# Fused attention, mixture of experts and MLP: the start and the end of the MLP rearranged

## The chip, the cores and the metric

One core of one Trainium2 chip. The metric is the device time of one execution, in microseconds (us); lower is better.

## The reference

Windowed and dilated attention, then a mixture of eight experts with one expert for each row, then an MLP whose activation is `h * cos(h)`. What is cut away here is the attention and the gate's softmax.

```python
def _moe_ref(x, expert_emb, tau, w1, w2):          # N = 2304, D = 512, E = 8, F = 1024
    ...                                            # expert_idx, gate_w: arg max and softmax of cosine logits
    for e in range(E):
        mask = expert_idx == e
        h = np.maximum(x[mask] @ w1[e], 0.0)
        out[mask] = gate_w[mask, None] * (h @ w2[e])

def _moe2_ref(x, w_in, w_out):                     # 512 -> 2048 -> 512
    h = x @ w_in
    g = h * np.cos(h)
    return (g @ w_out).astype(np.float32)
```

## The kernel before, in words

**Splitting.** Every matrix product of the experts and of the MLP is made of three passes (`passes`, L698): each operand is split into a high part, a rounded copy made by ScalarE, and a low part, the difference, made by VectorE, and TensorE adds high by low, low by high and high by high. So each weight tile costs ScalarE one copy (`weights_hi`, L912, L920) and VectorE one subtraction (`weights_lo`, L1222, L1227), and so do the input rows and the hidden layer.

**Experts.** The rows lie sorted by expert in `XS`; a block is up to 352 rows of one expert, with `nblk` blocks (8 with these inputs, at most 14). A block has eight units `f` (128 hidden columns each). For each unit TensorE does `expert_up(f)` (12 matmuls) and then `expert_dn` of two units before (12 matmuls), so units 6 and 7 of a block are brought down in the first units of the next (`expert_block`, L745). ScalarE's block (L978) takes each unit with a Relu (L986), converts weights of the next pair of units, at units 5 and 6 the next block's rows (L951), and at unit 6 the first pair of the next block's weights. Its `expert_dn_hi` at unit 6 waits until TensorE has done unit 5's down product, and unit 7's Relu stands behind it. In the last block (L1008 and L1397) that is skipped by an `If`. Blocks 0 to 5 are written out on all engines (`FLAT`); the rest are a `Fori` over pairs of blocks with an `If` for each (L766, L1017, L1408), which runs to block 13 and skips those that are not there. SyncE loads weights two pairs ahead (`load_expert`, L359), into two raw buffers for each of the two weights.

**Handing over to the MLP.** TensorE has left the loop and brings down units 6 and 7 of the last block, with `mlp_up(0, 0)` between them and `mlp_up(0, 1)` behind. SyncE waits until all expert weights are converted (L399) and then loads the first MLP weights (L407, L409). ScalarE converts `w_in` pair 0 as two halves, the input rows 0 to 383 in one instruction (`group_hi(0, 0)`, L1024, four row tiles of 128x384), `w_out` pair 0, rows 384 to 767, and then runs a Sin on two columns, which loads the sine table (L1076). VectorE makes the low parts in the same order (L1416 for rows). `mlp_up(m, i)` (L775) waits for the whole of the low rows. The rows buffers `yh`, `yl` share memory with the experts' `XS`.

**MLP.** Three groups `m` of 768 rows, each of two halves of 384; 32 units a group, a unit being one hidden tile `f` for one half; `unit_of` (L771) gives their order: two `f` of half 0, the same two of half 1. TensorE does `mlp_up(m, i)` (12 matmuls of 384 columns), then `mlp_dn(m, i - 2)` (9 of 512, into three banks for each half). Between them stands a chain over two engines: ScalarE `turns` (L1039), VectorE three steps (`reduce`, L1428 to L1433), ScalarE Abs and Sin (L1051, L1054), VectorE the gate (L1445), ScalarE the high part (L1045), VectorE the low part (`gated_lo`, L1438), which `mlp_dn` needs. At units 29 and 31 each engine also converts the rows of the next group's half 0 and half 1 in one instruction (L1024, L1416); on VectorE `group_lo` stands ahead of `gated_lo`. `group_out` (L1056, L1447) copies a half's three banks out (ScalarE the even ones, VectorE the odd ones) once the last down product of that half is done; half 0 at unit 31 behind the cosine or the gate, half 1 at unit 1 of the next group. GpSimd sends each copied tile to its rows of `out` by an indirect DMA (L526). The program ends when all have landed.

Of the kernel before, what the change touches and what calls it, by code (L numbers as in the profile page):

```python
# [5 lines left out]
ALU = mybir.AluOpType  # L6
# [7 lines left out]
P = 128  # L14
# [7 lines left out]
def fused_kernel(nc, q, k, v, emb, tau, w1, w2, w_in, w_out, out):  # L22
# [36 lines left out]
    FLAT = 6  # L59
    FIRST_INC = (1, 1, DT - 2)  # L60
    IDENT_STEPS, MASK_STEPS, CONSTS = 2, 6, 18
# [5 lines left out]
    with ExitStack() as ctx:  # L67
# [11 lines left out]
        half_pi = sb("half_pi", [P, 2])  # L79

# [157 lines left out]
        def weight_sems(p, units):  # L238

            return dict(  # L240
                up_in=[sem(f"{p}_up_in{i}") for i in range(2)], dn_in=[sem(f"{p}_dn_in{i}") for i in range(2)],
                up_hi=sem(f"{p}_up_hi"), up_lo=sem_from(f"{p}_up_lo", 2),
                dn_hi=sem(f"{p}_dn_hi"), dn_lo=sem_from(f"{p}_dn_lo", 2),
                up_mm=sem_from(f"{p}_up_mm", units), dn_mm=sem_from(f"{p}_dn_mm", units),
                in_hi=sem(f"{p}_in_hi"), in_lo=sem(f"{p}_in_lo"))
        ex = weight_sems("ex", 4)
        ml = weight_sems("ml", 8)
# [4 lines left out]
        table_loaded = sem("table_loaded")  # L252
        turns_ready = sem("turns_ready")
# [66 lines left out]
        def _(sp):  # L320
# [212 lines left out]
        def _(pe):  # L533
# [237 lines left out]
            def unit_of(i):  # L771

                return i // 4 * 2 + i % 2, i % 4 // 2

            def mlp_up(m, i):  # L775

                f, half = unit_of(i)
# [7 lines left out]
                for d in range(DT):  # L785
                    last = passes(bank[6 + i % 2][:, 0:HR], (up_h[s][:, d, cols], up_l[s][:, d, cols]),
                                  (yh[half][:, d, :], yl[half][:, d, :]), d == 0, d == DT - 1)
                last.then_inc(ml["up_mm"], 1)

            def mlp_dn(m, i):  # L790
# [6 lines left out]
                if i % 4 == 0:  # L797
                    pe.wait_ge(ml["dn_lo"], m * PAIRSTEPS2 + i // 4 + 3)
                i %= 2 * FT2
                f, half = unit_of(i)  # L800
                s = f // 2 % 2
                for c in range(3):
                    if f == 0:
# [5 lines left out]
                                  (dn_h[s][:, f % 2, :], dn_l[s][:, f % 2, :]), f == 0, f == FT2 - 1)  # L809
                last.then_inc(ml["dn_mm"], 1)  # L810
# [30 lines left out]
        def _(act):  # L841
# [136 lines left out]
            def expert_block(i, u, nblk):  # L978
# [3 lines left out]
                for f in range(FT):  # L982
# [73 lines left out]
            def group_out(m, half):  # L1056

                act.wait_ge(ml["dn_mm"], m * 2 * FT2 + (6 + 2 * half))
                act.wait_ge(o_free, m)
                for c in range(3 * half, 3 * half + 3):  # L1060
                    if c % 2 == 0:
# [10 lines left out]
            group_hi(0, 0)  # L1072
            act.wait_ge(ex["dn_mm"], nblk * FT + 2)
# [445 lines left out]
```

## Time and profile before

| | us |
|---|---|
| median of 3 runs | 874.77 (874.3 to 877.12) |
| the profiled execution, its own time | 870.1 |
| its span, first to last instruction | 868.4 |
| TensorE busy | 832.7 (96% of the span) |
| VectorE busy | 604.4 (70%) |
| ScalarE busy | 481.7 (55%) |
| TensorE's mean granted clock | 0.991 of full speed |

In the profile a step on TensorE appears as a matmul instruction with its start and modelled length; these lengths overlap, so the pace is read from one start to the next. "Idle before" in brackets is the time that the engine stood still before an instruction, with what ended it.

### The profile page before, as it was taken

The numbers are of one execution on the slowest core, as the hardware profiler recorded it, in microseconds if no ns is written. First come the engines' busy times: TensorE is split into PE (matmuls) and PEld (weight loads), VectorE is DVE, ScalarE is ACT, GpSimd is POOL, SyncE is SP. The second block draws the span as 40 slices with busy tenths as digits, with TensorE's granted clock in tenths as the row PEclk, the third lists the DMA queues.
The fourth block names the chain that finished last, engine by engine and source line by source line (L and its number), as shares of the span: only waits on it lengthen the run. The fifth ranks groups of instructions, "written<-read, shape, count | busy, mean of one in ns | idle before, by whom it ended". The sixth has DMA issues, their size and how long they took to land.

```text
span 868.4 us, 15558 instructions
## 1 busy us (share of the span) xinstructions
PE 832.7 (96%) x5034; PEld 757.4 (87%) x5034; DVE 604.4 (70%) x1157; ACT 481.7 (55%) x920; POOL 74.8 (9%) x129
## 2 busy tenths in 40 slices
PE   7999999979999999999989999999999999999993
PEld 6778876769999999999988999989999988999992
DVE  7888886676556556555567777788777788777762
ACT  4567764334445544454456665676666676566651
POOL 3112112141101000000000000002000002000002
PEclk9999999999999999999999999999999999999998
DMA  6597887035454343434242112113211214122001
GB/s 146 137 215 177 195 188 208 27 110 164 153 169 157 125 144 123 145 122 146 74 146 74 53 69 73 49 66 129 74 61 61 73 49 146 49 73 73 2 0 74
DMA packets 114912, 93.78 MB, mean 108 GB/s; under 512 B 65816, under 2 KB 94488, under 8 KB 114848
## 3 DMA queue, kind: packets, MB, share of 16 engines
q1 hardware_dynamic: 109920, 78.81, 31.4%
q0 software_dynamic: 4928, 14.16, 4.9%
q8 instruction: 35, 0.57, 0.3%
q14 instruction: 29, 0.24, 0.1%
HBM read 83.51 MB, written 9.44 MB: 107 GB/s over the span
## 4 chain that ended last, share of the span: by engine, by line
PE 83%; DVE 8%; ACT 2%; issue 2%; DMA 2%; POOL 1%; DVEq 0%; ACTq 0%; SPq 0%; POOLq 0%
PE bank L700 24%; PE bank L702 24%; PE bank L701 24%; PE bank L588 2%; PE bank L567 2%; PE bank L641 2%; PE bank L576 1%; PE bank L551 1%; DVE shifted L1168 1%; DVE row_max L1165 1%; DVE yl L1416 1%; ACT probs L869 1%; DMA xtok<-x_rows 1%; PE bank L657 1%; PE bank L742 1%
## 5 line engine op out<-in xcount | busy, mean ns | idle before, releaser
L700 PE MATMUL bank<-yh,up_l 128*128 128x384 f32 x384 | 129.7, 338 | 2.3 <-DVE yl L1416 2.3
L702 PE MATMUL bank<-yh,up_h 128*128 128x384 f32 x384 | 129.9, 338 | 0.0
L701 PE MATMUL bank<-yl,up_h 128*128 128x384 f32 x384 | 129.3, 337 | 0.0
L700 PE MATMUL bank<-dn_h,hid 128*128 128x512 f32 x288 | 112.7, 391 | 2.3 <-DVE hid L1438 1.8
L702 PE MATMUL bank<-dn_h,hid 128*128 128x512 f32 x288 | 113.9, 396 | 0.0
L701 PE MATMUL bank<-dn_l,hid 128*128 128x512 f32 x288 | 113.7, 395 | 0.0
L1227 DVE TENSOR_TENSOR dn_l<-dn_raw,dn_h 128x512 fp32r<-128x512 f32 (+1 forms) x80 | 71.9, 900 | 51.8 <-ACT dn_h L920 51.8
L1039 ACT ACTIVATE work<-bank 128x384 f32<-128x384 f32 x96 | 47.2, 492 | 80.4 <-PE bank L702 80.4
L700 PE MATMUL bank<-xh,up_l 128*128 128x352 f32 x256 | 83.9, 328 | 3.7 <-DVE up_l L1227 3.0
L1051 ACT ACTIVATE work<-work 128x384 f32<-128x384 f32 x96 | 50.4, 525 | 64.8 <-DVE work L1433 64.8
L1428 DVE TENSOR_SCALAR work<-work 128x384 f32<-128x384 f32 x96 | 34.5, 360 | 72.7 <-ACT work L1039 72.4
L920 ACT ACTIVATE dn_h<-dn_raw 128x512 fp32r<-128x512 f32 (+1 forms) x80 | 63.7, 798 | 37.7 <-PE bank L702 37.7
L700 PE MATMUL bank<-hid,dn_l 128*128 128x352 f32 x256 | 83.0, 324 | 0.8 <-issue 0.8
L701 PE MATMUL bank<-hid,dn_h 128*128 128x352 f32 x256 | 83.0, 324 | 0.0
L702 PE MATMUL bank<-hid,dn_h 128*128 128x352 f32 x256 | 82.6, 323 | 0.0
L702 PE MATMUL bank<-xh,up_h 128*128 128x352 f32 x256 | 82.3, 322 | 0.0
L701 PE MATMUL bank<-xl,up_h 128*128 128x352 f32 x256 | 82.0, 320 | 0.0
L1227 DVE TENSOR_TENSOR up_l<-up_raw,up_h 128x512 fp32r<-128x512 f32 (+1 forms) x80 | 71.9, 900 | 11.3 <-ACT up_h L920 10.7
L700 PEld LDWEIGHTS bank<-yh,up_l 128*128 128x128 f32 x384 | 72.3, 188 | 6.8 <-DVE yl L1416 2.6
L986 ACT ACTIVATE hid<-bank 128x352 fp32r<-128x352 f32 x64 | 29.7, 464 | 84.6 <-PE bank L702 84.2
L701 PEld LDWEIGHTS bank<-yl,up_h 128*128 128x128 f32 x384 | 72.3, 188 | 4.0
L702 PEld LDWEIGHTS bank<-yh,up_h 128*128 128x128 f32 x384 | 72.3, 188 | 0.0
(195 smaller groups left out, 1683.0 us busy)
## 6 DMA issues: line engine op xcount, KB each, us to landing
up_raw<-in_moe_w_dram SPq DMA_DIRECT2D x32, 512.0 KB, 3.6
dn_raw<-in_moe_w_dram SPq DMA_DIRECT2D x32, 512.0 KB, 3.5
up_raw<-in_moe_w_in_dram SPq DMA_DIRECT2D x24, 512.0 KB, 3.4
dn_raw<-in_moe_w_out_dram SPq DMA_DIRECT2D x24, 512.0 KB, 3.4
qn<-in_q_dram SPq DMA_DIRECT2D x32, 144.0 KB, 2.8
kn<-in_k_dram SPq DMA_DIRECT2D x32, 144.0 KB, 3.2
xtok<-x_rows SPq DMA_DIRECT2D x4, 1152.0 KB, 7.6
x_rows<-osb POOLq DMA_DIRECT2D x8, 288.0 KB, 3.6
```

Of the source, the lines that this page charges most:

```text
L567: last = mm(o[:QT, i * 256:(i + 1) * 256].rearrange("p (h c) -> p h c", h=2), qT[p % 2][:, t * QT:(t + 1) * QT], kT[p % 2][:, :, t * QT:t ...
L588: last = mm(bank[6 + s % 2][:QT, i * VN:(i + 1) * VN], probsT[s % 2][:, i * QT:(i + 1) * QT], vw[p % 2][:, 2 * u + i // 2, i % 2, :], star ...
L641: last = mm(bank[4 + G % 2][:E, 0:2 * QT], embT[:, d, :], xT[G % 2][:, d, :], start=d == 0, stop=d == DT - 1)
L700: mm(o, w[1], x[0], start=first, stop=False, skip_group_check=True)
L701: mm(o, w[0], x[1], start=False, stop=False, skip_group_check=True)
L702: return mm(o, w[0], x[0], start=False, stop=last, skip_group_check=True)
L920: A(hi[s][:, rows, :], raw[s][:, rows, :], ACT.Copy).then_inc(w[f"{which}_hi"], 1)
L986: A(hid[:, f % 4, 0, 0:TB], bank[4 + f % 4][:, 0:TB], ACT.Relu).then_inc(ex_h_hi, 1)
L1039: A(turns, bank[6 + i % 2][:, 0:HR], ACT.Copy, scale=1 / (2 * PI), bias=ROUND).then_inc(turns_ready, 1)
L1051: A(folded, red2, ACT.Abs).then_inc(folded_ready, 1)
L1227: ins = tt(lo[s][:, rows, :], raw[s][:, rows, :], hi[s][:, rows, :], ALU.subtract)
L1428: ts(whole, turns, ROUND, None, ALU.subtract).then_inc(whole_ready, 1)
```

## The change

The first pair of MLP weights is loaded and converted as if it belonged to the next expert (semaphores of `ex`), inside the last expert block. ScalarE and VectorE have all eight sure blocks written out, with the loop behind one `If(nblk > SURE)`. The first half's rows are converted in four pieces with a signal each. The sine table is loaded ahead of block 4. `group_lo` of later groups is split in two halves over units 29, 30, 31 and 0. In the last group the order of the last eight units is a list, and output tiles are signalled one by one (`chunk_mm`). SyncE's loop over groups is written out. The diff, cut to its core:

```diff
+    TRIG_BLOCK = 4
+    LAST_UNITS = ((12, 0), (13, 0), (12, 1), (14, 0), (15, 0), (13, 1), (14, 1), (15, 1))
...
-            sp.wait_ge(ex["up_lo"], nblk * PAIRSTEPS + 2)
-            sp.wait_ge(ex["dn_lo"], nblk * PAIRSTEPS + 2)
-            sp.sem_inc(carrier, 1)
...
-            with sp.Fori(0, NM) as m:
-                for j in range(PAIRSTEPS2):
+            for j in range(2):
+                sp.wait_ge(ex["up_lo"], nblk * PAIRSTEPS + (j + 1))
+                sp.dma_start(up_raw[j][:], win_v[:, :, 256 * j:256 * j + 256]).then_inc((ex, ml)[j]["up_in"][j], 16)
+                sp.wait_ge(ex["dn_lo"], nblk * PAIRSTEPS + (j + 1))
+                sp.dma_start(dn_raw[j][:], wout_v[:, 2 * j:2 * j + 2, :]).then_inc((ex, ml)[j]["dn_in"][j], 16)
+            sp.wait_ge(ex["up_lo"], nblk * PAIRSTEPS + 3)
+            sp.wait_ge(ex["dn_lo"], nblk * PAIRSTEPS + 3)
+            for m in range(NM):
+                for j in range(0 if m else 2, PAIRSTEPS2):
...
-            def unit_of(i):
+            def unit_of(m, i):
+                if m == NM - 1 and i >= 2 * FT2 - len(LAST_UNITS):
+                    return LAST_UNITS[i - 2 * FT2 + len(LAST_UNITS)]
                 return i // 4 * 2 + i % 2, i % 4 // 2
             def mlp_up(m, i):
...
-                if f == 0:
+                if f == 0 and (m, i) != (0, 0):
                     pe.wait_ge(ml["in_lo"], m * 2 + half + 1)
-                if i % 4 == 0:
-                    pe.wait_ge(ml["up_lo"], m * PAIRSTEPS2 + i // 4 + 3)
+                if (m, i) == (0, 0):
+                    pe.wait_ge(ex["up_lo"], nblk * PAIRSTEPS + 3)
+                elif f % 2 == 0:
+                    pe.wait_ge(ml["up_lo"], m * PAIRSTEPS2 + f // 2 + 3)
...
                 for d in range(DT):
+                    if (m, i) == (0, 0):
+                        pe.wait_ge(start_rows_lo, d + 1)
...
+                    if f == FT2 - 1 and c < 2:
+                        last.then_inc(chunk_mm, 1)
                 last.then_inc(ml["dn_mm"], 1)
...
                     elif f == FT - 2:
-                        if sure and b < SURE - 1:
-                            expert_up_hi(i, J)
-                            expert_dn_hi(i, J)
-                        else:
-                            with act.If(i * 2 + (u + 1) < nblk):
-                                expert_up_hi(i, J)
-                                expert_dn_hi(i, J)
+                        expert_up_hi(i, J)
+                        expert_dn_hi(i, J)
...
-            for b in range(1, FLAT):
+            for b in range(1, SURE):
+                if b == TRIG_BLOCK:
+                    A(trig_junk[:], half_pi[:], ACT.Sin).then_inc(trig_loaded, 1)
+                    act.wait_ge(trig_loaded, 1)
                 expert_block(b // 2, b % 2, nblk)
-            with act.Fori(FLAT // 2, NBLK // 2) as i:
-                for u in range(2):
-                    with act.If(i * 2 + u < nblk):
-                        expert_block(i, u, nblk)
+            with act.If(nblk > SURE):
+                with act.Fori(SURE // 2, NBLK // 2) as i:
...
             def group_out(m, half):
-                act.wait_ge(ml["dn_mm"], m * 2 * FT2 + (6 + 2 * half))
                 act.wait_ge(o_free, m)
                 for c in range(3 * half, 3 * half + 3):
+                    if c % 3 < 2:
+                        act.wait_ge(chunk_mm, (m - 1) * 4 + 2 * half + c % 3 + 1)
+                    else:
+                        act.wait_ge(ml["dn_mm"], m * 2 * FT2 + (6 + 2 * half - (m == NM and half == 0)))
                     if c % 2 == 0:
                         A(osb2[:, c, :], bank[c][:], ACT.Copy).then_inc(o_out_a, 1)
-            act.wait_ge(ex["up_lo"], nblk * PAIRSTEPS + 2)
-            act.wait_ge(ex["up_mm"], nblk * FT + 4)
-            whole_weights_hi("up", up_raw, up_h)
             act.wait_ge(y_out_a, nblk * 2)
             act.wait_ge(y_out_d, nblk * 2)
             act.wait_ge(ex["in_lo"], nblk * DT + DT)
-            group_hi(0, 0)
-            act.wait_ge(ex["dn_mm"], nblk * FT + 2)
-            whole_weights_hi("dn", dn_raw, dn_h)
+            for d in range(DT):
+                A(yh[0][:, d, :], X[:, d, 0:HR], ACT.Copy).then_inc(start_rows_hi, 1)
             group_hi(0, 1)
-            A(folded[:, 0:2], half_pi[:], ACT.Sin).then_inc(table_loaded, 1)
-            act.wait_ge(table_loaded, 2)
...
+                    if m == NM - 1 and i == 2 * FT2 - 1:
+                        group_out(NM, 0)
                     act_cosine(m, i)
...
-                    if i == 2 * FT2 - 1:
+                    if i == 2 * FT2 - 1 and m < NM - 1:
                         group_out(m + 1, 0)
...
-            for part in range(2):
-                weights_lo(ml, "up", up_raw, up_h, up_l, part + 1, 2, part)
-            group_lo(0, 0)
-            for part in range(2):
-                weights_lo(ml, "dn", dn_raw, dn_h, dn_l, part + 1, 2, part)
+            for d in range(DT):
+                dve.wait_ge(start_rows_hi, d + 1)
+                tt(yl[0][:, d, :], X[:, d, 0:HR], yh[0][:, d, :], ALU.subtract).then_inc(start_rows_lo, 1)
             group_lo(0, 1)
...
-                    if i in (2 * FT2 - 3, 2 * FT2 - 1):
-                        if m < NM - 1:
-                            group_lo(m + 1, (i - 2 * FT2 + 3) // 2)
+                    if i >= 2 * FT2 - 3 and m < NM - 1:
+                        group_lo(m + 1, (i - 2 * FT2 + 3) // 2, (i - 2 * FT2 + 3) % 2, 2)
+                    if i == 0 and m > 0:
+                        group_lo(m, 1, 1, 2)
```

VectorE's expert blocks, its `group_out` and the place of the last `group_out(NM, 0)` (ahead of `gate`) change as ScalarE's do.

## Rows read from the trace of the kernel before

**Rows 1.** The page: the span.

```profile
span 868.4 us, 15558 instructions
```

**Rows 2.** Waits of TensorE over the whole run: engine, line, releaser: us, times, longest.

```profile
PE bank L700 <- DVE yl L1416: 2.3, 1, 2.3
```

**Rows 3.** Timeline of TensorE, 408 to 457 us: start us, us, engine, line, op, operands.

```profile
409.49 0.32 PE L702 MATMUL bank<-hid,dn_h 128*128 128x352 f32 x1
...
440.11 0.32 PE L702 MATMUL bank<-hid,dn_h 128*128 128x352 f32 x1
...
441.21 0.42 PE L700 MATMUL bank<-hid,dn_l 128*128 128x352 f32 x1 [0.78 <-issue]
...
443.07 0.32 PE L702 MATMUL bank<-hid,dn_h 128*128 128x352 f32 x1
...
445.73 0.44 PE L700 MATMUL bank<-yh,up_l 128*128 128x384 f32 x1 [2.34 <-DVE yl L1416]
...
456.67 0.47 PE L700 MATMUL bank<-dn_h,hid 128*128 128x512 f32 x1 [0.94 <-DVE hid L1438]
```

**Rows 4.** Stretches: us, length, busy of each engine (instructions), PEclk, DMA share, GB/s.

```profile
194.00:196.00 2.00, 0.14 (x1) 0.14 (x2) 1.85 (x3) 0.95 (x2) 0.00 (x0) 1.00 0.00 0
...
447.00:448.00 1.00, 1.00 (x5) 1.00 (x4) 1.00 (x1) 0.80 (x2) 0.00 (x0) 0.50 0.04 12
```

**Rows 5.** Timeline of ScalarE, 318 to 447 us.

```profile
318.51 0.47 ACT L986 ACTIVATE hid<-bank 128x352 fp32r<-128x352 f32 x1 [0.45 <-PE bank L702]
...
409.91 1.06 ACT L920 ACTIVATE dn_h<-dn_raw 128x1024 fp32r<-128x1024 f32 x1 [3.62 <-PE bank L702]
...
410.88 0.45 ACT L986 ACTIVATE hid<-bank 128x352 fp32r<-128x352 f32 x1
...
441.36 1.15 ACT L920 ACTIVATE up_h<-up_raw 128x512 fp32r<-128x512 f32 x2 [2.34 <-issue]
...
446.32 1.28 ACT L1076 ACT_TABLE_LOAD   x1
```

**Rows 6.** Timeline of VectorE, 408 to 456 us.

```profile
412.14 0.95 DVE L1380 SCALAR_TENSOR_TENSOR hid<-bank,hid 128x352 fp32r<-128x352 f32 x2
...
426.31 1.23 DVE L1227 TENSOR_TENSOR dn_l<-dn_raw,dn_h 128x1024 fp32r<-128x1024 f32 x1 [2.04 <-ACT dn_h L920]
...
446.80 1.75 DVE L1416 TENSOR_TENSOR yl<-X,yh 128x1536 fp32r<-128x1536 f32 x1
...
449.49 0.36 DVE L1428 TENSOR_SCALAR work<-work 128x384 f32<-128x384 f32 x1 [0.94 <-ACT work L1039]
...
454.21 0.36 DVE L1428 TENSOR_SCALAR work<-work 128x384 f32<-128x384 f32 x1 [0.52 <-ACT work L1039]
```

**Rows 7.** Timeline of TensorE and VectorE, units 27 of group 0 to 1 of group 1.

```profile
565.60 0.39 PE L700 MATMUL bank<-dn_h,hid 128*128 128x512 f32 x1
...
569.79 0.39 PE L700 MATMUL bank<-dn_h,hid 128*128 128x512 f32 x1
...
571.97 1.75 DVE L1416 TENSOR_TENSOR yl<-X,yh 128x1536 fp32r<-128x1536 f32 x1
...
591.44 0.39 PE L700 MATMUL bank<-dn_h,hid 128*128 128x512 f32 x1
```

**Rows 8.** Timeline of TensorE, VectorE and GpSimd, the last output tiles.

```profile
853.02 0.50 PE L700 MATMUL bank<-dn_h,hid 128*128 128x512 f32 x1 [0.36 <-DVE hid L1438]
...
855.40 1.29 DVE L1453 COPY osb<-bank 128x512 f32<-128x512 f32 x2 [2.43 <-PE bank L702]
...
856.37 0.97 POOL L526 DMA_INDIRECT out_dram<-osb,id_now  x1 [1.09 <-DVE osb L1453]
...
858.92 0.97 POOL L526 DMA_INDIRECT out_dram<-osb,id_now  x1 [0.30 <-issue]
```

**Rows 9.** The page: a queue's packets, MB, share; an issue's count, KB, us to landing.

```profile
q8 instruction: 35, 0.57, 0.3%
...
dn_raw<-in_moe_w_out_dram SPq DMA_DIRECT2D x24, 512.0 KB, 3.4
```

More of the change, by code:

```diff
@@ L236, in fused_kernel, with weight_sems @@
         carrier = sem("carrier")
-        def weight_sems(p, units):
+        def weight_sems(p, units, rows=0):
+            if not rows:
+                pairs = dict(up_in=[sem(f"{p}_up_in{i}") for i in range(2)], dn_in=[sem(f"{p}_dn_in{i}") for i in range(2)],
+                             up_hi=sem(f"{p}_up_hi"), up_lo=sem_from(f"{p}_up_lo", 2),
+                             dn_hi=sem(f"{p}_dn_hi"), dn_lo=sem_from(f"{p}_dn_lo", 2))
+            else:
+                pairs = dict(up_in=[sem_from(f"{p}_up_in0", 16), sem(f"{p}_up_in1")],
+                             dn_in=[sem_from(f"{p}_dn_in0", 16), sem(f"{p}_dn_in1")],
+                             up_hi=sem_from(f"{p}_up_hi", 2), up_lo=sem_from(f"{p}_up_lo", 3),
+                             dn_hi=sem_from(f"{p}_dn_hi", 2), dn_lo=sem_from(f"{p}_dn_lo", 3))
             return dict(
-                up_in=[sem(f"{p}_up_in{i}") for i in range(2)], dn_in=[sem(f"{p}_dn_in{i}") for i in range(2)],
-                up_hi=sem(f"{p}_up_hi"), up_lo=sem_from(f"{p}_up_lo", 2),
-                dn_hi=sem(f"{p}_dn_hi"), dn_lo=sem_from(f"{p}_dn_lo", 2),
+                **pairs,
                 up_mm=sem_from(f"{p}_up_mm", units), dn_mm=sem_from(f"{p}_dn_mm", units),
-                in_hi=sem(f"{p}_in_hi"), in_lo=sem(f"{p}_in_lo"))
+                in_hi=sem_from(f"{p}_in_hi", rows) if rows else sem(f"{p}_in_hi"),
+                in_lo=sem_from(f"{p}_in_lo", rows) if rows else sem(f"{p}_in_lo"))
         ex = weight_sems("ex", 4)
-        ml = weight_sems("ml", 8)
+        ml = weight_sems("ml", 8, 1)
+        start_rows_hi = sem("start_rows_hi")
+        start_rows_lo = sem("start_rows_lo")
+        chunk_mm = sem("chunk_mm")
         ex_h_hi = sem("ex_h_hi")
@@ L252, in fused_kernel @@
         table_loaded = sem("table_loaded")
+        trig_loaded = sem("trig_loaded")
         turns_ready = sem("turns_ready")
@@ L1392, in expert_block @@
                     elif f == FT - 2:
-                        if sure and b < SURE - 1:
-                            expert_up_lo(i, J)
-                            expert_dn_lo(i, J)
-                        else:
-                            with dve.If(i * 2 + (u + 1) < nblk):
-                                expert_up_lo(i, J)
-                                expert_dn_lo(i, J)
+                        expert_up_lo(i, J)
+                        expert_dn_lo(i, J)
                     if sure and tile_at(b, f) is not None:
@@ L1405, in _, with group_lo @@
             last_start = dve.value_load(table[0:1, 1, bass.ds(nblk, 1)], min_val=0, max_val=N)
-            for b in range(FLAT):
+            for b in range(SURE):
                 expert_block(b // 2, b % 2, nblk)
-            with dve.Fori(FLAT // 2, NBLK // 2) as i:
-                for u in range(2):
-                    with dve.If(i * 2 + u < nblk):
-                        expert_block(i, u, nblk)
-            def group_lo(m, half):
+            with dve.If(nblk > SURE):
+                with dve.Fori(SURE // 2, NBLK // 2) as i:
+                    for u in range(2):
+                        with dve.If(i * 2 + u < nblk):
+                            expert_block(i, u, nblk)
+            def group_lo(m, half, part=0, parts=1):
                 dve.wait_ge(ml["in_hi"], m * 2 + half + 1)
-                tt(yl[half][:], X[:, :, bass.ds(m * MR + half * HR, HR)], yh[half][:], ALU.subtract).then_inc(ml["in_lo"], 1)
+                ds_ = slice(part * DT // parts, (part + 1) * DT // parts)
+                ins = tt(yl[half][:, ds_, :], X[:, ds_, bass.ds(m * MR + half * HR, HR)], yh[half][:, ds_, :], ALU.subtract)
+                if part == parts - 1:
+                    ins.then_inc(ml["in_lo"], 1)
             def mlp_weights_lo(m, i):
@@ L1483, in _ @@
                             mlp_weights_lo(m, i)
+                    if m == NM - 1 and i == 2 * FT2 - 1:
+                        group_out(NM, 0)
                     gate(m, i)
@@ L1489, in _ @@
                         before_this(dve, m, lambda: group_out(m, 1))
-                    if i == 2 * FT2 - 1:
+                    if i == 2 * FT2 - 1 and m < NM - 1:
                         group_out(m + 1, 0)
```

20 lines of the change are left out of this document (15 added, 5 removed).

## The prediction

> **What bounds the kernel now.** I read the page first: the span is 868.4 us [rows 1], and TensorE is the engine that is busy nearly throughout, so only time in which it stands still, or runs slower, can be won. The profiled execution took 870.1 us, 1.7 more than its span; the median of the runs shown is 874.77, so 4.7 more than the execution that I reason from. What those 4.7 are, no row tells. I take differences from the profile and set them on the median.
>
> Then the view of TensorE's waits: the longest inside the MLP is for the low rows `yl`, 2.3 us, once [rows 2]. The timeline of TensorE shows the place, the hand-over from the last expert block to the MLP [rows 3]. The last matmul of block 7's down unit 5 starts at 440.11; unit 6 starts at 441.21 (0.78 idle, "issue": the loop's skipped blocks); it is through at about 443.23 (443.07 and a pace of 0.16); `mlp_up(0, 0)` starts at 445.73, behind a wait for `yl`; `mlp_dn(0, 0)` starts at 456.67, behind another 0.94 for the low part of the hidden layer. In between TensorE fell from 2.4 to 1.2 GHz: granted clock 0.50 from 447 to 448 [rows 4]. That loss is in the pace of the matmuls, not in a wait. A stretch of 2 us with 0.14 us of matmuls (194 to 196) kept 1.00 [rows 4], so idle time here does not always bring the clock down.
>
> Next, why `yl` was late. ScalarE's next step behind its last Relu began at 441.36, after 2.34 us of "issue" [rows 5]: it ran through three passes of the loop with six tests, all not taken. Only then came weights, rows, weights, rows, and the table load at 446.32, 1.28 long [rows 5]. VectorE followed it: second row instruction at 446.80 (1.75), first step of the first unit at 449.49, first step of the second at 454.21, of which 0.52 was a wait that goes back to TensorE's half clock [rows 6].
>
> Two more places. The start of the down products runs at 4.19 us a unit (565.60 to 569.79), but from 565.60 to 591.44 six units take 25.84, where six times 4.19 are 25.14 [rows 7]: 0.70 lost at the border of two groups, where VectorE has the 1.75 us of `yl` (571.97) ahead of `gated_lo`. The other border has the same pattern, so there are two. And the end: last down unit from 853.02, first copy of half 1 at 855.40, the last three scatters at 856.37 to 858.92, one each 1.27 (0.97 and 0.30 of issue), then 8.5 us to the end of the span [rows 8].
>
> **The change, part by part. Hand-over.** SyncE's loads of MLP pair 0 move ahead: `w_out` pair 0 waits for the low part of pair 2 of block 7, which ends at 427.54 (426.31 + 1.23) [rows 6], and lands 3.4 later [rows 9], about 431. Its loads are queued behind each other as an expert's are, and nothing else stands behind them. ScalarE now converts `up` pair 0 in the slack of unit 6, and `dn` pair 0 when unit 5's down product is done; the Relu of unit 7 is queued behind that. Block 6 shows how long this takes: last matmul of unit 5 at 409.49, conversion 409.91, Relu 410.88 [rows 3, 5], VectorE's low part of unit 7 as the first of a pair from 412.14 (0.95 for two, so 0.48 a step) [rows 6]. Set on 440.11 this gives conversion 440.53, Relu 441.50 to 441.95, low part 442.76 to about 443.25. So the Relu waits for a conversion that the old last block did not have, but unit 7's down product is not started before `mlp_up(0, 0)` is over, so TensorE does not feel it.
>
> Behind it stand one test and branch over the loop on each engine. No row shows it alone. Bounds: 0, since VectorE ran two Relu halves of different blocks back to back across such a test at 412.14 [rows 6]; and 2.34, the whole loop on ScalarE [rows 5]. I take 0.4, that is 2.34 / 6. The first low row tile then runs from 443.65 to 444.2, and `mlp_up(0, 0)` starts at 444.3, not 445.73: 1.4 earlier. It needs a tile each 0.52 us (three matmuls), VectorE gives one each 0.48, so the four signals cost nothing after the first.
>
> But TensorE is not what sets the end of this stretch; VectorE's chain is. Four tiles end at 445.6, the rows of half 1 take 1.7, and the first step of unit 0 starts at about 447.3 (before: 449.49), 2.2 earlier. `mlp_up(0, 0)` is over by 446.4, in time. From there the chain to `mlp_dn(0, 0)` is the old one, less the 0.52 of waiting for half-clock matmuls, if the clock stays: 2.7 earlier at 456.67. **Term 1: 2.7 us**, bounds 1.2 (half clock again, or a slow branch) and 3.4 (branch free). I expect the clock to stay, because the idle time between unit 6 and `mlp_up` falls from 2.5 to about 1 us. The 0.78 of TensorE's own loop stays.
>
> **Sine table.** 1.28 and a short Sin move from 446.32 to the front of block 4. There ScalarE stood idle 0.45 before the Relu at 318.51 [rows 5], so that Relu and the weight copy behind it come about 1.1 late. The hidden unit is needed two units, some 7.6 us, later, the weights one unit pair later, so this costs nothing; without that cover it would be 1.1. What it saves is in term 1: at the new pace ScalarE would be in the load when `turns` is due. After the load at 446.32 Copy and Abs ran with no second load; no row shows a Relu behind a sine load. The Trainium skill, "ScalarE: Activation LUTs", section "Table sets: the hidden batching unit", says that relu, copy and abs are in every set as filler; by it no further load comes.
>
> **Written-out blocks.** ScalarE and VectorE have slack in blocks 6 and 7 and TensorE's loop is unchanged: nothing gained but the loop's 2.34, counted above. The unrolled SyncE loop issues the same loads: nothing.
>
> **Borders.** `yl` in halves: 0.85 instead of 1.7 ahead of `gated_lo` at units 29 to 31 and 0. The low part of unit 28 then ends about 0.85 before its old time, and TensorE lost only half of the 0.70 there. At unit 0 the half instruction is new, but `gated_lo` of unit 31 is due a whole product later than it can be done. **Term 2: 2 x 0.70, of which I take 1.3**; bounds 0 and 1.4.
>
> **Tail.** With the new list half 0 finishes one unit earlier and is copied ahead of the last cosine, so its three scatters leave by about 853.3. The last gate no longer has ScalarE's two copies between it and the high part: the last down unit starts up to 0.2 earlier, 852.8. Its first third is done at about 853.8, the copy 0.7 later at 854.5, the scatters at 854.8, 856.0 and 857.3 instead of 858.92. The three issues at 1.27 are the limit, and the 8.5 us behind the last remain. The weights for the moved unit (14, 0) are converted at unit 25, three units before it. **Term 3: 1.6 us**; bounds 0.5 and 1.8.
>
> Sum: 2.7 + 1.3 + 1.6 = 5.6. On the profiled execution 870.1 - 5.6 = 864.5; on the median 874.77 - 5.6 = 869.2.
>
> **Rivals.**
> (a) The hand-over gives only 1.2: the branch costs up to 2.34, or the clock falls again, since the stretch still has 0.9 us of issue and about 1 of wait. For it: the fall at 447 came behind two such gaps. Against it: 194 to 196. Total 1.2 + 1.3 + 1.6 = 4.1, so 870.7. One form of it is an instruction fetch behind the jump. The instruction queue moved 35 packets in 0.3% of 16 engines' span [rows 9], 1.2 us each (0.003 x 16 x 868.4 / 35), so a fetch costs at least that. The Trainium skill, "Runtime: NRT & Kernel Launch", section "Instruction fetch mechanics", says that a taken branch to a target outside the pages held forces a fetch before execution goes on; no row here shows one alone.
> (b) Borders and tail give little (another wait takes their place: `yl` of half 1 at unit 0 delays `gated_lo`, or the landing of the last scatter is what ends, not its issue). Then 2.7 + 0 + 0.5 = 3.2, so 871.6; together with (a) 1.7, so 873.1, which is no measurable difference.
> (c) Slower: `w_out` pair 0 comes late. ScalarE's Relu of unit 7 is now queued behind that conversion, so each us after 440.5 is a us of the chain. It decides only if the load lands more than 9 us after the 431 above; to end 2.6 slower it must be some 17 us late. Against it: 24 such loads took 3.4 in the median. Some 877.5.
> (d) The change does nothing at the hand-over because TensorE was bound by its own loop: excluded by the wait for `yl` in rows 2.
>
> **How the numbers follow.** Forecast 0.66, (a) 0.13, (b) 0.12, both together 0.06, (c) 0.03. The forecast's own range is 867.9 to 870.9 (terms at 6.9 and 3.9); 8 in 10 with the median's spread of some 1.5 us gives 866.6 to 872.8. About 0.3%, 2.6 us, is what a measurement of this kernel can tell from no change: faster means below 872.15. Faster: the forecast, (a) and 0.07 of (b), 0.86; same 0.10, the rest of (b) and nearly all of both together; slower 0.04.
>
> **What would show it.** In the changed profile: no 2.34 of issue on ScalarE at the hand-over; `mlp_up(0, 0)` about 1 us after unit 6; granted clock 1.00 from 440 to 460; the table load near 318 with no wait on TensorE behind it; seven down starts over each border at 25.1; last scatter 1.6 earlier to the last gate, and 8.5 us behind it unchanged. Wrong would be: a clock of 0.50 after 444, a second table load, a wait of TensorE for `hid` at the borders, or a longer stretch behind the last scatter.

## The result and the profile after

The changed kernel took 870.60 us (median of 8 runs, 867.19 to 871.85), the kernel before 874.82 on the same chip; the ratio of the fast runs is 0.9938 (95% interval 0.9919 to 0.9957), which stands for 5.4 us, while the two medians lie 4.2 apart. Timed twice more the ratio came to 0.9916 (0.9898 to 0.9935) and 0.9925 (0.9897 to 0.9953). So it is faster, by 4 to 7 us according to the first interval and by up to 9 according to the others. The forecast was 869.2, within 866.6 to 872.8.

The profiled execution took 867.19 us, 2.9 less than the one before. From the page, its span and the busy time of the engines ("to [rows 1]" names the rows of the kernel before that it is to be read against):

```profile
span 865.2 us, 15473 instructions
...
PE 832.7 (96%) x5034; PEld 756.8 (87%) x5034; DVE 604.9 (70%) x1162; ACT 481.7 (56%) x921; POOL 75.9 (9%) x129
```

TensorE's work is the same 832.7 us. Its waits, longest in total first, a choice (to [rows 2]):

```profile
PE bank L719 <- DVE xl L1386: 3.3, 1, 3.3
...
PE bank L719 <- DVE hid L1464: 1.4, 3, 0.6
...
PE bank L719 <- issue: 0.8, 1, 0.8
...
PE bank L719 <- DVE yl L1486: 0.5, 1, 0.5
```

`yl` at the hand-over has fallen from 2.3 to 0.5 us. The 3.3 us for `xl` is in the start of the first expert block and was 0.7 before; it belongs to a stretch that the change does not touch, and the experiments come back to it.

**Hand-over.** TensorE, ScalarE (with the moved table load) and VectorE, in three fences (to [rows 3, 5, 6]):

```profile
442.69 0.32 PE L721 MATMUL bank<-hid,dn_h 128*128 128x352 f32 x1
...
443.79 0.42 PE L719 MATMUL bank<-hid,dn_l 128*128 128x352 f32 x1 [0.78 <-issue]
...
446.47 0.41 PE L719 MATMUL bank<-yh,up_l 128*128 128x384 f32 x1 [0.49 <-DVE yl L1486]
...
455.82 0.47 PE L719 MATMUL bank<-dn_h,hid 128*128 128x512 f32 x1 [0.63 <-DVE hid L1464]
```

```profile
320.66 1.28 ACT L1041 ACT_TABLE_LOAD   x1
...
322.19 0.46 ACT L1015 ACTIVATE hid<-bank 128x352 fp32r<-128x352 f32 x1
...
443.11 1.06 ACT L949 ACTIVATE dn_h<-dn_raw 128x1024 fp32r<-128x1024 f32 x1 [3.62 <-PE bank L721]
...
444.07 0.45 ACT L1015 ACTIVATE hid<-bank 128x352 fp32r<-128x352 f32 x1
...
444.42 1.75 ACT L1101 ACTIVATE yh<-X 128x384 fp32r<-128x384 f32 x4
...
448.83 0.49 ACT L1067 ACTIVATE work<-bank 128x384 f32<-128x384 f32 x1 [1.28 <-PE bank L721]
```

```profile
445.34 0.52 DVE L1407 SCALAR_TENSOR_TENSOR hid<-bank,hid 128x352 fp32r<-128x352 f32 x1
...
445.77 1.96 DVE L1486 TENSOR_TENSOR yl<-X,yh 128x384 fp32r<-128x384 f32 x4
...
449.35 0.36 DVE L1454 TENSOR_SCALAR work<-work 128x384 f32<-128x384 f32 x1
```

ScalarE goes from its last Relu (444.07) into the row tiles (444.42) with no "issue" between, and VectorE from its last low part (445.34) into `yl` (445.77). `mlp_up(0, 0)` starts 3.78 us after the last matmul of block 7's down unit 5, not 5.62, and `mlp_dn(0, 0)` 13.13 after it (442.69 to 455.82), not 16.56. The table load stands ahead of block 4's first Relu, which runs right behind it without another load. The 20 us around the hand-over have the full clock (the column PEclk, third from the end):

```profile
440.00:460.00 20.00, 18.06 (x100) 16.56 (x100) 15.36 (x27) 12.43 (x23) 0.00 (x0) 1.00 0.27 91
```

**Border of two groups.** TensorE's down units 27 and 33 of the MLP (568.92 and 594.33), and up unit 0 and down unit 31 between them (to [rows 7]); then VectorE:

```profile
568.92 0.39 PE L719 MATMUL bank<-dn_h,hid 128*128 128x512 f32 x1
...
583.56 0.33 PE L719 MATMUL bank<-yh,up_l 128*128 128x384 f32 x1
...
585.86 0.50 PE L719 MATMUL bank<-dn_h,hid 128*128 128x512 f32 x1
...
594.33 0.39 PE L719 MATMUL bank<-dn_h,hid 128*128 128x512 f32 x1
```

```profile
584.39 0.95 DVE L1440 TENSOR_TENSOR yl<-X,yh 128x768 fp32r<-128x768 f32 x1
...
585.25 0.55 DVE L1464 TENSOR_TENSOR hid<-work,hid 128x384 fp32r<-128x384 f32 x1
```

Six units take 25.41 us, not 25.83. Six undisturbed ones take 25.14, so 0.27 is left, and it comes from one place: up unit 0 of the new group starts at 583.56 and its twelve matmuls take 2.09, but down unit 31 begins only at 585.86, behind the low part that VectorE wrote from 585.25 to 585.80, and that stood behind the half of `yl` at 584.39.

**Tail.** Last down unit, first copy of half 1, first and last of its three scatters (to [rows 8]):

```profile
851.10 0.50 PE L719 MATMUL bank<-dn_h,hid 128*128 128x512 f32 x1 [0.18 <-DVE hid L1464]
...
852.16 0.69 DVE L1482 COPY osb<-bank 128x512 f32<-128x512 f32 x1 [1.12 <-issue]
...
853.13 0.97 POOL L545 DMA_INDIRECT out_dram<-osb,id_now  x1 [1.24 <-DVE osb L1482]
...
855.69 0.97 POOL L545 DMA_INDIRECT out_dram<-osb,id_now  x1 [0.30 <-issue]
```

The copy starts 1.06 us after the unit, where it was 2.38 before, and the last scatter is at 855.69, 3.5 after that copy in both kernels; 9.5 us to the end of the span behind it, as before.

### The profile page after: what moved, and what is told of

It is laid out like the page before. It is cut to its first block, busy times and chain, and to the rows that moved or that the text cites. A ratio compares the mean times of both kernels' runs of the same rounds, so it can differ in the third digit from the quotient of the medians.

```text
span 865.2 us, 15473 instructions
## 1 busy us (share of the span) xinstructions
PE 832.7 (96%) x5034; PEld 756.8 (87%) x5034; DVE 604.9 (70%) x1162; ACT 481.7 (56%) x921; POOL 75.9 (9%) x129
## 4 chain that ended last, share of the span: by engine, by line
PE 84%; DVE 7%; issue 2%; ACT 2%; DMA 2%; POOL 1%; another core or an unknown queue 0%; DVEq 0%; ACTq 0%; POOLq 0%; SPq 0%
PE bank L721 24%; PE bank L719 24%; PE bank L720 24%; PE bank L607 2%; PE bank L586 2%; PE bank L660 2%; PE bank L595 1%; PE bank L570 1%; DVE shifted L1195 1%; DVE row_max L1192 1%; ACT probs L898 1%; PE bank L676 1%; DMA xtok<-x_rows 1%; DVE kT L319 1%; PE bank L761 1%
```

## Experiments

In all of them I measure three stretches from TensorE's starts in the timeline: the **hand-over**, from the last matmul of block 7's down unit 5 to the first of `mlp_dn(0, 0)`; a **border**, from down unit 27 of a group to down unit 1 of the next (six units), two of them; and the **tail**, from down unit 29 of the last group to the end of the span. The last column is when the hand-over begins. us:

| run | hand-over | borders | tail | begins at |
|---|---|---|---|---|
| before | 16.56 | 25.83, 25.82 | 20.88 | 440.11 |
| e0, before again | 16.48 | 25.86, 25.85 | 20.89 | 448.36 |
| after | 13.13 | 25.41, 25.37 | 19.43 | 442.69 |
| e1, after again | 13.13 | 25.41, 25.36 | 19.43 | 443.97 |
| e8, after, third | 13.13 | 25.41, 25.34 | 19.37 | 442.26 |
| e2, borders whole | 13.13 | 25.85, 25.84 | 19.44 | 446.46 |
| e5, loops back | 15.07 | 25.38, 25.36 | 19.42 | 445.58 |
| e6, sine late | 13.56 | 25.41, 25.36 | 19.42 | 443.49 |
| e7, rows whole | 14.56 | 25.42, 25.36 | 19.40 | 444.48 |
| e3, tail by halves | 13.13 | 25.42, 25.36 | 20.82 | 444.77 |
| e4, tail old | 13.15 | 25.40, 25.36 | 21.04 | 446.25 |
| v8, w_out later | 12.38 | 25.42, 25.36 | 19.37 | 443.19 |
| v9, TensorE's branch | 13.85 | 25.41, 25.36 | 19.46 | 442.03 |
| v12, all | 13.94 | 25.12, 25.12 | 19.42 | 445.01 |

A stretch that an edit does not touch repeats within 0.1 us, while the times of whole executions differ by several us; so parts of 0.4 to 3 us can be told apart here by single profiles. Where a run is named by one time, it is one execution beside one or a few of the kernel before.

**e0, e1, e8: both kernels again.** No edit.

> The kernel before, unchanged, for its profile. Both theories: from the last matmul of block 7's down unit 5 to the first of mlp_dn(0, 0) 16.6 us, six units over a border 25.8, from the start of down unit 29 of the last group to the end 20.9. What is open is the stretch ahead of the experts. Theory: the changed kernel's first expert matmul at 191.47 instead of 188.84 was chance (ScalarE and GpSimd both saw a signal of TensorE 2.7 us late), so the first expert matmul of single runs of either kernel lies anywhere from 188.5 to 192. Rival: the change shifts it, and this one is at 189 again.

> The changed kernel, unchanged. Theory: the three stretches as in its first profile (13.1, 25.4, 19.4 us, against 16.6, 25.8 and 20.9 before), together 5.8 us, and a ratio near 0.9935. Ahead of the experts it is not behind the kernel before by a fixed amount. Rival: the change costs some 2 us ahead of the experts in each run, first expert matmul at 191 or later, which takes back a part of the 5.8, so that the ratio stays near 0.996.

> The changed kernel once more, timed beside v12 on one chip. Both theories: 13.1, 25.4 and 19.4 us in the three stretches, a ratio of 0.991 to 0.994; v12 is under it by 2 us (theory) or by less than 1 (rival).

e0 took 878.86 us; e1 868.38 (median of 5; ratio 0.9916) and e8 866.30 (median of 6; ratio 0.9925). The three stretches came out as in the first profiles. What differs is ahead of them. The first expert matmul starts at 188.84 and 194.87 in the two profiles of the kernel before (e0 thus lies beyond the 188.5 to 192 that was expected) and at 191.47, 189.91 and 188.76 in the three of the changed one, so the changed kernel is not the later one. TensorE's wait for `xl` there is 0.72 in both profiles of the kernel before and 3.31, 1.15 and 0.72 in the changed one, so it varies between executions of one kernel. The hand-over begins at 440.11 and 448.36 in the two profiles of the kernel before and at 442.26 to 443.97 in three of the changed one. The stretches of 20 us around the start of the experts show a good part of it in the clock, column PEclk. e0, with the stretch of the hand-over behind:

```profile
180.00:200.00 20.00, 16.43 (x116) 15.78 (x114) 10.62 (x35) 6.04 (x11) 9.06 (x9) 0.79 0.41 119
...
200.00:220.00 20.00, 18.14 (x107) 18.07 (x108) 10.71 (x14) 7.66 (x13) 4.13 (x4) 0.91 0.53 160
...
440.00:460.00 20.00, 16.90 (x94) 16.33 (x93) 11.91 (x18) 11.00 (x18) 0.00 (x0) 0.91 0.48 159
```

e0 lost 0.21 and 0.09 of 20 us each there, 6 us of full clock; the first profile of the kernel before had 0.98 and 1.00 in the same two stretches, e1 0.92 and 0.99. So the 2.6 us by which the first profile of the changed kernel was behind at the hand-over are within the spread of one and the same kernel; a fixed cost of the change ahead of the experts (the rival) is not seen: the ratio did not stay near 0.996.

**e2: `group_lo` whole at the borders.**

```diff
-                    if i >= 2 * FT2 - 3 and m < NM - 1:
-                        group_lo(m + 1, (i - 2 * FT2 + 3) // 2, (i - 2 * FT2 + 3) % 2, 2)
-                    if i == 0 and m > 0:
-                        group_lo(m, 1, 1, 2)
+                    if i in (2 * FT2 - 3, 2 * FT2 - 1) and m < NM - 1:
+                        group_lo(m + 1, (i - 2 * FT2 + 3) // 2)
```

> VectorE's group_lo in one instruction at units 29 and 31 again, all else as changed. Theory: only the borders move, back from 25.4 to 25.8 us for six units, twice, so 0.85 us longer in all; hand-over 13.1 and tail 19.4 stay. Rival: the borders gained by the other weights and outputs order, and stay at 25.4.

The borders went back to 25.85 and 25.84, the rest stayed. The split alone carries the borders' gain, 0.44 and 0.48 us.

**e5: blocks 6 and 7 in the loop again on ScalarE and VectorE.**

```diff
-            with act.If(nblk > SURE):
-                with act.Fori(SURE // 2, NBLK // 2) as i:
+            with act.Fori(FLAT // 2, NBLK // 2) as i:
...
-            for b in range(1, SURE):
+            for b in range(1, FLAT):
```

and the same on VectorE.

> ScalarE and VectorE have blocks 6 and 7 in the loop again, with no test around it; the weights of MLP pair 0 are still converted in block 7. Theory: ScalarE stands 2.3 us behind its last Relu, the first row tile comes that much later, mlp_up(0, 0) starts some 2.0 us later than in the changed kernel, and the hand-over is 1.5 to 2.3 longer (14.6 to 15.4 us). Rival: the branches are hidden behind the instructions that the engine still has in its queue, as at a test between two blocks, and the hand-over stays at 13.1 to 13.4.

ScalarE stands 1.53 us between its last Relu and the first row tile, not the 2.3 expected (the first fence: its timeline), VectorE 1.83 between its last low part and its first row tile (the second), and `mlp_up(0, 0)` waits 2.42 (the third: TensorE's):

```profile
446.97 0.45 ACT L1015 ACTIVATE hid<-bank 128x352 fp32r<-128x352 f32 x1
...
448.94 1.76 ACT L1100 ACTIVATE yh<-X 128x384 fp32r<-128x384 f32 x4 [1.53 <-issue]
```

```profile
448.23 0.52 DVE L1406 SCALAR_TENSOR_TENSOR hid<-bank,hid 128x352 fp32r<-128x352 f32 x1
...
450.59 1.97 DVE L1484 TENSOR_TENSOR yl<-X,yh 128x384 fp32r<-128x384 f32 x4 [1.83 <-ACT yh L1100]
```

```profile
451.29 0.41 PE L719 MATMUL bank<-yh,up_l 128*128 128x384 f32 x1 [2.42 <-DVE yl L1484]
```

VectorE's wait is put down to ScalarE, but ScalarE's first row tile, one of four in 1.76 us, was over by about 449.5, 1.1 us before VectorE began. So it is mostly VectorE's own loop that holds it: its first row tile starts 5.01 us after the hand-over's start mark (445.58), 1.93 later than in the changed kernel (3.08), and ScalarE's only 1.63 later.

The hand-over is 15.07, 1.94 longer than with the loops behind one test. So the passes through blocks that are not there were on the path, and the one test that replaced them costs nothing that shows. One more thing: with idle pieces of 0.78 and 2.42 us, as long as before, the clock stayed at 1.00 here:

```profile
440.00:460.00 20.00, 16.77 (x98) 15.62 (x96) 13.64 (x23) 11.15 (x21) 0.00 (x0) 1.00 0.24 79
```

It did so in e7 too, where the pieces were 0.76 and 1.95. Both profiles of the kernel before fell to 0.91 in that stretch (e0 above).

**e6: the sine table behind the rows again.**

```diff
-                if b == TRIG_BLOCK:
-                    A(trig_junk[:], half_pi[:], ACT.Sin).then_inc(trig_loaded, 1)
-                    act.wait_ge(trig_loaded, 1)
...
             group_hi(0, 1)
+            A(trig_junk[:], half_pi[:], ACT.Sin).then_inc(trig_loaded, 1)
+            act.wait_ge(trig_loaded, 1)
```

> The sine table is loaded behind the rows of half 1 again, as before, and not at block 4; all else as changed. Theory: ScalarE is free at about 447.55 in the changed kernel's profile and the first turns starts at 448.83, so of the 1.5 us of load and Sin only 0.25 is late, and the hand-over is 13.3 to 13.5 us instead of 13.13. Rival: the load stands on the path and costs its whole 1.3 to 1.5 (14.4 to 14.6). At block 4 neither expects a wait of TensorE in the changed kernel.

ScalarE's timeline:

```profile
448.37 1.28 ACT L1100 ACT_TABLE_LOAD   x1
...
450.05 0.49 ACT L1064 ACTIVATE work<-bank 128x384 f32<-128x384 f32 x1 [0.18 <-ACT trig_junk L1100]
```

`turns` starts at 450.05, 6.56 after the hand-over begins, where the changed kernel has 6.14 (448.83 after 442.69). The hand-over is 13.56: the move is worth 0.43 us here, not the 0.25 expected, since the Sin and its wait end later than I had set, and by far not the whole 1.5.

**e7: rows of half 0 in one piece.**

```diff
-            for d in range(DT):
-                A(yh[0][:, d, :], X[:, d, 0:HR], ACT.Copy).then_inc(start_rows_hi, 1)
+            A(yh[0][:], X[:, :, 0:HR], ACT.Copy).then_inc(start_rows_hi, DT)
...
-            for d in range(DT):
-                dve.wait_ge(start_rows_hi, d + 1)
-                tt(yl[0][:, d, :], X[:, d, 0:HR], yh[0][:, d, :], ALU.subtract).then_inc(start_rows_lo, 1)
+            dve.wait_ge(start_rows_hi, DT)
+            tt(yl[0][:], X[:, :, 0:HR], yh[0][:], ALU.subtract).then_inc(start_rows_lo, DT)
```

> The rows of half 0 are converted in one instruction on each engine, with one signal; all else as changed. Theory: mlp_up(0, 0) waits for 1.47 and 1.75 us instead of two pieces, starts 1.2 to 1.3 later, and since in the changed kernel VectorE's first step ends its wait only just after the rows of half 1, that moves the whole chain: hand-over 14.2 to 14.5 us. Rival: VectorE's chain of low parts is the path and has the same work (a bit less) in one piece: 13.0 to 13.4.

VectorE's timeline, the whole of `yl` and the first step of unit 0:

```profile
447.78 1.76 DVE L1484 TENSOR_TENSOR yl<-X,yh 128x1536 fp32r<-128x1536 f32 x1
...
452.56 0.36 DVE L1453 TENSOR_SCALAR work<-work 128x384 f32<-128x384 f32 x1 [1.36 <-ACT work L1067]
```

14.56, just over the expected range. VectorE does less work than with four pieces and then stands 1.36 us: it is `mlp_up(0, 0)`, which could not start on the first tile, that is late. The rival is out. The four signals are worth 1.43.

**e3, e4: the tail.** e3 waits for the half's last down product on both engines and keeps the order of units and the early `group_out`; e4 has order, waits and place as before.

```diff
-                    if c % 3 < 2:
-                        act.wait_ge(chunk_mm, (m - 1) * 4 + 2 * half + c % 3 + 1)
-                    else:
-                        act.wait_ge(ml["dn_mm"], m * 2 * FT2 + (6 + 2 * half - (m == NM and half == 0)))
+                    act.wait_ge(ml["dn_mm"], m * 2 * FT2 + (6 + 2 * half - (m == NM and half == 0)))
```

> The changed kernel, but each output tile waits for the last down product of its whole half, not of itself; the new order of units and the early group_out stay. Theory: the signals for single tiles carry the gain: the three last scatters start after the whole last unit again, and from down unit 29 of the last group to the end it is 20.7 to 20.9 us, against 19.43 changed and 20.88 before. Rival: the new order carries it, since it takes the first three scatters out of the way: 19.5 to 20.0.

> The changed kernel with order, waits and place of the outputs of the last group as before. Both theories: from down unit 29 to the end 20.9 us, hand-over 13.1 and borders 25.4 as changed. If it is under 20.7, something else of the change shortens the tail.

Copy and scatters of half 1 in e3 (VectorE, then GpSimd):

```profile
855.67 1.29 DVE L1476 COPY osb<-bank 128x512 f32<-128x512 f32 x2 [2.53 <-PE bank L721]
...
856.64 0.97 POOL L545 DMA_INDIRECT out_dram<-osb,id_now  x1 [2.65 <-DVE osb L1476]
...
859.19 0.97 POOL L545 DMA_INDIRECT out_dram<-osb,id_now  x1 [0.30 <-issue]
```

20.82 and 21.04. The signals for single tiles carry 1.39 of the 1.45; order and place without them gave 0.06 against the kernel before (0.22 against e4). The order does what it was meant to: in e3 the last down unit starts 5.32 us after unit 29 (847.88 to 853.20), in the changed kernel 5.33, in the kernel before 5.50 and in e4 5.57. But in e3 and e4 the first copy starts 2.47 and 2.45 after that unit, not 2.38, and this takes a part back. e4 is 0.16 longer than the kernel before itself, 0.07 ahead of the last down unit and 0.07 between it and the copy; why, stays open.

**v8: `w_out` pair 0 behind the start rows**, beyond the changed kernel:

```diff
                         expert_up_hi(i, J)
-                        expert_dn_hi(i, J)
+                        if not (sure and b == SURE - 1):
+                            expert_dn_hi(i, J)
...
             with act.If(nblk > SURE):
+                expert_dn_hi(SURE // 2 - 1, 2 * PAIRSTEPS)
...
             group_hi(0, 1)
+            with act.If(nblk < SURE + 1):
+                expert_dn_hi(SURE // 2 - 1, 2 * PAIRSTEPS)
```

and the same on VectorE.

> Beyond the changed kernel: w_out pair 0 is converted behind the start rows, not ahead of the last Relu, so that the Relu no longer waits behind it. Theory (that queue sets when the row tiles start): ScalarE's Relu comes right after block 7's last up product, some 3 us earlier, mlp_up(0, 0) starts with no wait behind down unit 6 (3.1 us after the last matmul of unit 5, not 3.78), VectorE's first step some 0.7 earlier, and the hand-over is 12.3 to 12.5 us. Rival: the conversion, moved into VectorE's chain, costs there what it saves: 13.0 to 13.8.

ScalarE's last Relu, first row tile and first `turns`, and TensorE's `mlp_up(0, 0)`:

```profile
441.61 0.47 ACT L1015 ACTIVATE hid<-bank 128x352 fp32r<-128x352 f32 x1 [1.67 <-PE bank L721]
...
442.28 1.76 ACT L1103 ACTIVATE yh<-X 128x384 fp32r<-128x384 f32 x4 [0.21 <-issue]
...
448.57 0.49 ACT L1069 ACTIVATE work<-bank 128x384 f32<-128x384 f32 x1 [2.20 <-PE bank L721]
```

```profile
446.29 0.34 PE L719 MATMUL bank<-yh,up_l 128*128 128x384 f32 x1
```

The Relu runs 1.58 us before the hand-over's start mark (443.19), not 1.38 behind it, `mlp_up(0, 0)` follows down unit 6 with no wait (3.10 after the mark), and the hand-over is 12.38, within the range given. So in the changed kernel the conversion ahead of the Relu does set when the row tiles start. One execution took 866.70.

**v9: TensorE's blocks written out too**, and **v12: v8, v9 and a border edit**:

```diff
-            for b in range(1, FLAT):
+            for b in range(1, SURE):
                 expert_block(b // 2, b % 2)
-            with pe.Fori(FLAT // 2, NBLK // 2) as i:
+            with pe.If(nblk > SURE):
+                with pe.Fori(SURE // 2, NBLK // 2) as i:
```

v12 also has, on VectorE, `gated_lo` ahead of the second half of the low rows at unit 0:

```diff
-                    if i == 0 and m > 0:
-                        group_lo(m, 1, 1, 2)
                     if i >= 1:
                         gated_lo(m, i - 1)
                     else:
                         before_this(dve, m, lambda: gated_lo(m, -1))
+                    if i == 0 and m > 0:
+                        group_lo(m, 1, 1, 2)
```

> Beyond the changed kernel: TensorE too has blocks 6 and 7 written out and one test around its loop, so that its 0.78 us of issue goes. Theory: nothing is won, since mlp_up(0, 0) waits for VectorE's first row tile: the wait before it grows from 0.49 to about 1.2 and the hand-over stays at 13.0 to 13.2 us. Rival: TensorE's loop is a part of the path, 12.3 to 12.6.

> Both together, and at the borders the second half of the low rows of half 1 stands behind gated_lo of unit 31. Theory: with the row tiles early, TensorE's issue now counts: hand-over 11.4 to 11.8 us; and the wait of down unit 31 goes, six units over a border at 25.1 to 25.2 instead of 25.4; together 1.9 to 2.2 us under the changed kernel and a ratio near 0.990 to the kernel before. Rival: another wait holds the hand-over at 12.3 or more, and the border stays at 25.4 since unit 0 has the same work in another order.

TensorE's timeline, `dn` unit 6 and `mlp_up(0, 0)`, of v9; VectorE's first row tiles of v9; TensorE's of v12; and v12's instruction queue from its page:

```profile
443.24 0.42 PE L719 MATMUL bank<-hid,dn_l 128*128 128x352 f32 x1 [0.89 <-issue]
...
446.60 0.34 PE L719 MATMUL bank<-yh,up_l 128*128 128x384 f32 x1 [1.18 <-DVE yl L1487]
```

```profile
445.11 1.95 DVE L1487 TENSOR_TENSOR yl<-X,yh 128x384 fp32r<-128x384 f32 x4
```

```profile
446.40 0.43 PE L719 MATMUL bank<-hid,dn_l 128*128 128x352 f32 x1 [1.06 <-issue]
...
449.68 0.33 PE L719 MATMUL bank<-yh,up_l 128*128 128x384 f32 x1 [1.09 <-issue]
```

```profile
q8 instruction: 37, 0.61, 0.3%
```

Neither expectation held for v9 (867.04 us in its one execution): the issue before unit 6 grew from 0.78 to 0.89, and the hand-over from 13.13 to 13.85. The wait before `mlp_up(0, 0)` reads 1.18, as expected, but it isn't VectorE's: the row tiles start 3.08 after the mark (442.03) as in the changed kernel, where `mlp_up(0, 0)` follows 3.78 after the mark and here only 4.57. So some 0.8 us of it is TensorE's own. In v12 the issue before unit 6 is 1.06, and another 1.09 us of issue stands ahead of `mlp_up(0, 0)`, which waits for nothing else: 13.94 where v8 alone had 12.38. On TensorE the jump over the written-out loop costs more than running through it. Both kernels moved 37 instruction packets, the changed one 35; their code is also longer by two blocks on TensorE, so the packets alone do not show where TensorE waited. The border edit did what was expected: 25.12 twice, no loss left (six times 4.19 is 25.14). As a whole v12 took 869.35 (median of 8), ratio 0.9948 (0.9927 to 0.9969), beside e8's 0.9925 on the same chip: no improvement. By the stretches it should be 0.3 behind e8 (0.81 more, 0.29 and 0.22 less); the rest of the 3 us between the medians is, in the two profiled executions, ahead of the hand-over (it begins at 445.01 and 442.26), and whether v12 has a part in that was not tried. The version that the stretches point to, v8 with the border edit and TensorE's loop as it is, has not been run.

## Why the prediction was right, and where a step was off

The sum was 5.6 us; the three stretches give 3.43 + 0.42 + 0.45 + 1.45 = 5.75 in the first pair of profiles, and the three ratios 5.4, 7.4 and 6.6 of 875 (the medians 4.2, 6.8 and 6.5). The size of the sum is thus right, by three terms of which two were mis-sized in opposite directions; that 0.7 too little and 0.4 too much nearly cancel is luck.

**Term 1, hand-over: 3.4 measured (3.43, 3.35 against e0), 2.7 predicted,** at its upper bound. The step that was off is "I take 0.4, that is 2.34 / 6" for the test and branch. The lower bound, 0, was right: VectorE went from its last low part to the first row tile in 0.43 us, the normal pace. Its first step on unit 0 came 6.66 us after the mark (449.35 after 442.69) and not 7.19, which is 0.53 of the 0.73; the other 0.2 lies behind that step, where the wait that went was larger than the 0.52 counted (see the clock, below). The rest of the working held: the Relu of unit 7 behind the conversion of `w_out` (1.38 after the mark, 1.39 worked out), VectorE's low part at 2.65 after it as in block 6, and VectorE's chain as what sets the end. e5 shows the loops as the largest part (1.94), e7 the four signals (1.43), e6 the sine table (0.43); each is undone alone, so they need not add up to the 3.43, and the earlier conversion of `w_in` pair 0 was not undone by itself. The prediction gave the four signals no value of their own; they are needed because in one piece TensorE, not VectorE, becomes the late one. All three are differences at the same full clock.

**The clock** stayed full, as forecast, in all twelve profiles with the changed hand-over. The reason I gave, shorter idle time, is not shown: e5 had idle pieces as long as before (0.78 and 2.42) and kept the clock too. What brought it down in both profiles of the kernel before stays open.

Its share in the gain is larger than the 0.52 us that the prediction counted. In the kernel before, VectorE's first step too waited 0.94 [rows 6], for a `turns` that stood behind the slow matmuls of `mlp_up(0, 0)` (the first fence: ScalarE's timeline of the kernel before); in e0, where the clock fell earlier, it waited 1.51 (the second: VectorE's):

```profile
448.97 0.49 ACT L1039 ACTIVATE work<-bank 128x384 f32<-128x384 f32 x1 [1.15 <-PE bank L702]
```

```profile
458.30 0.36 DVE L1428 TENSOR_SCALAR work<-work 128x384 f32<-128x384 f32 x1 [1.51 <-ACT work L1039]
```

An estimate of the kernel before at the full clock: `mlp_up(0, 0)` starts 5.62 after the mark as it did; from there to `turns` it is 2.36 in the changed kernel (446.47 to 448.83), from `turns` to VectorE's first step 0.52 (448.97 to 449.49), and from that step to `mlp_dn(0, 0)` 6.47 (449.35 to 455.82). That makes 14.97, not 16.56. So about 1.6 of the 3.4 us go with the clock and 1.8 with the rearranged work. No run has the old work at the full clock, so this split is worked out and not measured. The prediction had the absolute time of the chain nearly right all the same, since it let `mlp_up(0, 0)` run at the full clock.

**Term 2, borders: 0.87 measured, 1.3 predicted.** The step that failed: "at unit 0 the half instruction is new, but `gated_lo` of unit 31 is due a whole product later than it can be done". It was due at 585.65 and done at 585.80. The border had lost about 0.35 at each of two places; the first loss went whole, of the second 0.27 stayed. v12, with the two exchanged, shows that this was all of the remaining loss.

**Term 3, tail: 1.45 measured, 1.6 predicted.** The working held to 0.15. The order of units moved the last down unit by 0.17 (5.33 after unit 29, not 5.50), where "up to 0.2" was predicted, and the signals did the rest; the last scatter stands 4.59 behind that unit's start, where 4.5 was worked out. That the three issues at 1.27 are the limit is right: 3.5 us from the first copy of half 1 to the last scatter in both kernels, and 9.5 from that scatter's start to the end (8.5 from its end, as in the prediction).

**Costs set at nothing.** Sine table in block 4: TensorE has no wait between 315 and 440 us. The Relu behind it came at 322.19 without a further load; the Trainium skill, "ScalarE: Activation LUTs", section "Table sets: the hidden batching unit", has relu in every set, and the trace agrees: two loads in the whole run. Rival (c), a late `w_out`: the load was issued at 430.14, such loads land 3.5 later by the page's median, and the conversion waited for TensorE alone until 443.11, so there were some 9 us to spare.

**Rival (a)**, a fetch behind the jump, did not come about on ScalarE and VectorE, but v9 and v12 met something like it on TensorE. The Trainium skill, "Runtime: NRT & Kernel Launch", section "Instruction fetch mechanics", says that a taken branch to a target outside the two pages held forces a fetch before execution goes on; by it, a jump over TensorE's two blocks (384 matmuls and as many weight loads) would pay and one over ScalarE's few dozen instructions might not. The trace agrees as far as it goes (0.89 and about 0.8 in v9, 1.06 and 1.09 in v12; 0 on the other two engines). Each of these gaps is below the 1.2 that the prediction gave as the least price of a fetch, and the first replaces the loop's 0.78. Which packet ended which wait, no view shows, so a fetch as the cause is not shown.

## What to carry to other kernels

When one engine is busy 96% of the time, look at each gap for the chain that ends it and mark the stretch by two starts on the busy engine: such a stretch repeats within 0.1 us, where whole runs differ by several. A signal for each tile pays where the consumer takes tiles in order (first row tile, last output tile: 1.4 us each here), an instruction of 1.7 us in front of a short one on the path costs its overhang until it is split and set behind it. A loop over work that is not there is worth putting behind one test (1.94 us here on ScalarE and VectorE together), but try it on each engine by itself: on TensorE it cost 0.72. And where the clock falls in a stretch, work out what the old order would take at the full clock before crediting the whole gain to the edit.

## What was not expected of the hardware

A test and jump over a loop of two blocks took no time that shows on ScalarE and VectorE (0.43 us from one VectorE instruction to the next, the normal pace), and 0.1 to 0.3 us more than the loop itself on TensorE, with a second gap one unit later, of about 0.8 us in v9 and 1.09 in v12. And TensorE's clock: after 0.78 and 2.42 us of idle time it stayed at full speed in e5, while both profiles of the kernel before, with 0.78 or 0.76 and 2.34, had 0.91 in the 20 us around.
